# Alpha's products taken for two units at once, the first loads, scores and low halves in another order: a fused linear-attention and two-MoE kernel on one core

## The reference

```python
def _attn_ref(q, k, v, alpha):                 # (4, 8, 768, 48) each
    for t in range(S):
        state = alpha[:, :, t, :, None] * state + np.einsum('bhd,bhe->bhde', k[:, :, t], v[:, :, t])
        y[:, :, t] = np.einsum('bhd,bhde->bhe', q[:, :, t], state)

x = attn_out.transpose(0, 2, 1, 3).reshape(3072, 384)
h = x @ w_in1;  x = (h * (1.0 / (1.0 + np.exp(-1.702 * h)))) @ w_out1     # 384 -> 2048 -> 384
h = x @ w_in2;  x = (h - np.tanh(h)) @ w_out2
```

## Time and profile before

| what | value |
|---|---|
| median of 3 runs | 967.76 us (967.51 to 970.03) |
| profiled execution | 967.3 us, its span 965.5 us |
| PE busy | 943.8 us (98%) |
| DVE busy | 672.2 us (70%) |
| ACT, POOL busy | 376.4 us (39%), 285.4 us (30%) |
| granted TensorE clock | 1.00 in every stretch looked at |

### The profile page before, as it was taken

The page is one execution under the profiler, slowest core; times in us unless marked ns, Lnnn a source line. Parts: engine busy times, 40 slices in busy tenths (PEclk is TensorE's granted clock), DMA queues, the critical chain, the costliest instruction groups (busy, mean ns, idle before and its releaser), DMA issues.

```text
span 965.5 us, 23370 instructions
## 1 busy us (share of the span) xinstructions
PE 943.8 (98%) x9705; PEld 830.0 (86%) x9705; DVE 672.2 (70%) x1615; ACT 376.4 (39%) x730; POOL 285.4 (30%) x314
## 2 busy tenths in 40 slices
PE   5899999999999999999999999999999999999998
PEld 4789999999999988888888888888888888888886
DVE  7879997878888877776322544357677677776765
ACT  1352333332332332333234664244444444444442
POOL 2666665646556554444001642000000000000000
PEclk9999999999999999999999999999999999999999
DMA  7943232423323332321113322010020020100101
GB/s 156 256 89 91 49 86 51 114 49 85 80 61 83 90 69 47 104 47 25 19 58 123 98 82 90 1 37 30 1 66 2 1 66 1 40 27 1 34 1 33
DMA packets 136234, 58.94 MB, mean 61 GB/s; under 512 B 114368, under 2 KB 131520, under 8 KB 136128
## 3 DMA queue, kind: packets, MB, share of 16 engines
q1 hardware_dynamic: 133488, 55.39, 22.8%
q10 hardware_dynamic: 2640, 2.05, 0.7%
HBM read 43.26 MB, written 13.96 MB: 59 GB/s over the span
## 4 chain that ended last, share of the span: by engine, by line
PE 92%; DVE 3%; DMA 2%; SPq 1%; POOL 1%; issue 1%; ACT 0%; DVEq 0%; POOLq 0%; ACTq 0%
PE pX L840 39%; PE pZ L864 16%; PE pX L864 9%; PE pZ L908 6%; PE pZ L914 6%; PE pX L908 4%; PE pX L704 3%; PE pZ L799 2%; PE pZ L732 2%; PE pZ L690 1%; PE pZ L742 1%; DMA k<-k_t 1%; PE pX L835 1%; PE pX L718 1%; PE pZ L790 1%; DVE scores L1212 1%
## 5 line engine op out<-in xcount | busy, mean ns | idle before, releaser
L840 PE MATMUL pX<-x_hi,w_hi 128*128 128x512 f32 (+2 forms) x624 | 227.7, 365 | 0.7 <-ACT g L1050 0.7
L840 PE MATMUL pX<-x_lo,w_hi 128*128 128x512 f32 (+2 forms) x624 | 227.3, 364 | 0.0
L840 PE MATMUL pX<-x_hi,w_lo 128*128 128x512 f32 (+2 forms) x624 | 227.3, 364 | 0.0
L1228 DVE TENSOR_TENSOR g_lo<-g,g_hi 128x512 fp32r<-128x512 f32 (+2 forms) x208 | 129.3, 637 | 87.5 <-ACT g_hi L1059 87.3
L1059 ACT ACTIVATE g_hi<-g 128x512 fp32r<-128x512 f32 (+2 forms) x208 | 121.3, 583 | 89.5 <-DVE g L1308 85.9
L1050 ACT ACTIVATE g<-pX 128x512 f32<-128x512 f32 (+3 forms) x144 | 65.7, 456 | 206.4 <-PE pX L840 173.2
L1308 DVE TENSOR_TENSOR g<-pX,sg 128x512 f32<-128x512 f32 x96 | 66.3, 690 | 106.2 <-ACT sg L1052 106.2
L840 PEld LDWEIGHTS pX<-x_hi,w_hi 128*128 128x128 f32 x624 | 117.5, 188 | 18.0 <-ACT g L1050 1.1
L840 PEld LDWEIGHTS pX<-x_lo,w_hi 128*128 128x128 f32 x624 | 117.5, 188 | 16.9
L840 PEld LDWEIGHTS pX<-x_hi,w_lo 128*128 128x128 f32 x624 | 117.5, 188 | 16.8
L596 POOL TENSOR_TENSOR r<-r,alpha 112x128 f32<-112x128 f32 (+2 forms) x115 | 109.5, 968 | 18.5 <-DMA r<-q_t 14.9
(11 more groups left out here) (166 smaller groups left out, 1899.4 us busy)
## 6 DMA issues: line engine op xcount, KB each, us to landing
v<-v_l SPq DMA_DIRECT2D x96, 48.0 KB, 2.6
x_raw<-hidden SPq DMA_DIRECT2D x6, 768.0 KB, 5.7
attn_out<-y SPq DMA_DIRECT2D x92, 48.0 KB, 1.8
out_t<-o SPq DMA_DIRECT2D x10, 384.0 KB, 3.5
alpha<-a_t SPq DMA_DIRECT2D x24, 128.0 KB, 2.9
r<-q_t SPq DMA_DIRECT2D x24, 128.0 KB, 3.0
k<-k_t SPq DMA_DIRECT2D x24, 128.0 KB, 3.0
w_raw<-w_in SPq DMA_DIRECT2D x16, 192.0 KB, 2.4
```

The costliest lines, as they stand in the source:

```text
L840: last = nc.tensor.matmul(pH(N)[:, 0:w], win(wp, f, m), XS[T % 2][xp][:, m, 0:w], start=(n == 0), stop=(n == len(terms) - 1))
L1228: nc.vector.tensor_tensor(at(GLs, N), g_raw(N), at(GHs, N).bitcast(F32), ALU.subtract).then_inc(gl_done, 1)
```

## The change

It does the following.

- Alpha, SF1, T4, T16, F4, F16 and T64 hold two units side by side. `product_step` now does units 1 and 2, then 3 and 4, and so on in one pass (12 instructions of twice the size; unit 0 and, at the end, 23 alone), and `ahead` skips the alpha steps at every second odd item. Alpha's loads have a semaphore for each buffer and SP issues two units' alpha at once.
- In the opening, SP issues unit 1's alpha before the masks and unit 2's alpha before v of unit 0; ACT issues the g = 0 weights only after unit 1's q has landed; `first_inputs` is dealt out differently between SP and ACT, both starting with the first copy of y; ACT's `plain_queries(1)` comes after them. Unit 2's q and k go before both g = 1 weights; the g = 3 out weights go after unit 3's q and k. `first_unit` does alpha's first eight steps before any query. One warm-up product fewer.
- The up products 1 and 3 write bank O0 instead of H0, so a product need not wait for the gelu of the one before it, and the first `down` waits until four gelus are through (`g_done` 4) and the first states are copied.
- Visits stand at 0, 5, 9, 13, 17, 21, 25, 30, 33, 36, 40, 44, 47, 50, ... instead of 0, 4, 8, 12, 16, 20, 25, 30, 33, 36, 39, 42, 45, 49, 52, 55, 58, 61, ...; both lists go on with 64. Below N = 32 `plain_queries` comes after the visit's copies, not one N before.
- The low halves of w_out are one a period from N = 30 to 45. `x_low(2)` stands in the visit at N = 25, before its `ahead`.

```diff
 def batch_of(U):        return (U + 1) // 2
 def batch_end(U):       return min(2 * batch_of(U), UNITS - 1) + 1
...
-    starts = ([0, 4, 8, 12, 16, 20, 25, 30] + [33 + 3 * n for n in range(5)] + [49 + 3 * n for n in range(5)]
+    starts = ([0, 5, 9, 13, 17, 21, 25, 30, 33, 36, 40, 44, 47, 50, 53, 55, 58, 61]
...
 X_AT = {1: 13, 3: 12}
+XLOW_AT = {1: 9}
...
         def pH(N):
+            if N in (1, 3):
+                return O0
             return H0 if N < L1B * NF or N % 2 == 0 else H1
...
             def load_alpha(U):
-                if U:
-                    sp.wait_ge(t_step, (U - 1) * T_STEPS + T_AL)
-                    sp.wait_ge(q_step, (U - 1) * Q_STEPS + Q_AL)
+                if U > 1:
+                    sp.wait_ge(t_step, batch_of(U - 2) * T_STEPS + T_AL)
+                    sp.wait_ge(q_step, (U - 2) * Q_STEPS + Q_AL)
...
             load_k(sp, 0, 0)
+            load_alpha(1)
             sp.dma_start(MASK[:], masks).then_inc(mask_loaded, 16)
+            load_qk(1)
+            load_alpha(2)
             load_v(0)
-            load_alpha(1)
-            load_qk(1)
...
+                if U == 2:
+                    load_w(sp, 3, slice(1, 2))
                 if U == 1:
                     sp.wait_ge(y_copied, 1)
-                    first_inputs(sp, ((0, 0), (0, 1), (1, 0), (1, 1)))
+                    first_inputs(sp, ((0, 0), (1, 0)))
                 sp.wait_ge(y_copied, 2 * U)
                 if U == 1:
-                    first_inputs(sp, ((2, 0), (3, 0)))
+                    first_inputs(sp, ((2, 1), (3, 1)))
...
                 if U == 1:
-                    load_alpha(2)
-                    load_w(sp, 1, slice(1))
                     load_qk(2)
-                    load_w(sp, 1, slice(1, 2))
+                    load_w(sp, 1)
...
-                if U + 2 < UNITS:
-                    load_alpha(U + 2)
+                for W in (U + 2, U + 3):
+                    if U % 2 and W < UNITS:
+                        load_alpha(W)
                 if U == 1:
-                    load_w(sp, 3)
+                    load_w(sp, 3, slice(1))
...
                 if N < L1N:
-                    if N:
-                        pe.wait_ge(g_done, N)
+                    if N > 1:
+                        pe.wait_ge(g_done, N if N > 4 else N - 1)
...
                 if T < PLAIN:
-                    pe.wait_ge(g_done, N + 1)
+                    pe.wait_ge(g_done, max(4, N + 1))
...
+                if N == 0:
+                    pe.wait_ge(state_step, states_before(LEAD))
...
             plain_queries(0)
+            act.wait_ge(q_loaded[1], 32)
             load_w(act, 0)
-            plain_queries(1)
             copy_outputs(0)
+            act.wait_ge(y_copied, 1)
+            first_inputs(act, ((0, 1), (1, 1)))
             copy_outputs(1)
             act.wait_ge(y_copied, 2)
-            first_inputs(act, ((2, 1), (3, 1)))
+            first_inputs(act, ((2, 0), (3, 0)))
+            plain_queries(1)
...
-            queries_at = {VISIT_OF[j + 1] - 1: j // 2 + 1 for j in range(LEAD, ITEMS - 2, 2)}
+            queries_at = {VISIT_OF[j + 1] - (VISIT_OF[j + 1] >= L1P): j // 2 + 1 for j in range(LEAD, ITEMS - 2, 2)}
...
                 U = (j + 3) // 2 if j % 2 else j // 2 + 1
-                if U >= UNITS:
+                if U >= UNITS or j % 2 and U % 2 == 0:
                     return
...
             late = {NF + 1 + F: [(0, F)] for F in range(NF)}
-            for F in range(10):
-                late[NF + 6 + F].append((1, F))
-            late.update({2 * NF + 1: [(1, 10), (1, 11)], 2 * NF + 2: [(1, 12), (1, 13)], 2 * NF + 4: [(1, 14), (1, 15)]})
+            for F in range(NF):
+                late.setdefault(2 * NF - 2 + F, []).append((1, F))
...
                         states(j)
+                        if XLOW_AT.get(T) == f:
+                            x_low(T + 1)
                         ahead(j, 0)
```

More of the change, by code:

```diff
@@ L110, in made, with batch_of, batch_end @@
     return item_of(j)[3] < CHUNKS - 1
+def batch_of(U):
+    return (U + 1) // 2
+def batch_end(U):
+    return min(2 * batch_of(U), UNITS - 1) + 1
 def keys_before(j):
@@ L243, in build @@
         V = [sb(f"v_{u}", [P, 2, QP, D], where=att) for u in U2]
-        T64 = [sb(f"t64_{u}", [PX, SL], where=att) for u in U2]
+        T64 = sb("t64", [PX, 2 * SL], where=att)
         Y = [sb(f"y_{u}", [PX, 2, QP, C], where=att) for u in U2]
[L246 to L251, removed]
+        AL = sb("alpha", [PX, 2 * SL, C], where=att)
+        SF1 = sb("sf1", [PX, 2 * SL, C], where=att)
+        T4 = sb("t4", [PX, 2 * SL, 4, 4], where=att)
+        T16 = sb("t16", [PX, 2 * SL, 4], where=att)
+        F4 = sb("f4", [PX, 2 * SL, 8, 4], where=att)
+        F16 = sb("f16", [PX, 2 * SL, 8], where=att)
         S = sb("state", [PX, 2, SL, D], where=att)
@@ L376, in load_rows, with part_of, alpha_count @@
                 eng.dma_start(part, rows[at:at + (HS, D)[h]]).then_inc(done, 16)
+        def part_of(U):
+            n = (U + 1) % 2
+            return slice(n * SL, (n + 1) * SL)
+        def alpha_count(U):
+            return 32 * batch_of(U)
         def load_a(eng, U, half=None):
-            load_rows(eng, AL[:].rearrange("p (s t) -> p s t", s=SL), aT, U, al_loaded, half)
+            load_rows(eng, AL[:, part_of(U), :], aT, U, al_loaded[U % 2] if U else al0_loaded, half)
         def load_q(eng, U, half=None):
@@ L1049, in _ @@
                 if T < L1B:
-                    nc.scalar.activation(g_raw(N), H0[:, 0:width(T)], ACT.Gelu_apprx_sigmoid).then_inc(g_done, 1)
+                    nc.scalar.activation(g_raw(N), pH(N)[:, 0:width(T)], ACT.Gelu_apprx_sigmoid).then_inc(g_done, 1)
                 else:
@@ L1097, in product_step @@
             def product_step(U, s):
-                a, sf1 = ([t[:].rearrange("p (c s b) -> p c s b", s=4, b=16)[:, :, d, :] for d in range(4)]
-                          for t in (AL, SF1))
+                both = slice(part_of(U).start, part_of(batch_end(U) - 1).stop)
+                a, sf1 = ([t[:, both, d * 16:(d + 1) * 16] for d in range(4)] for t in (AL, SF1))
+                t4, f4 = T4[:, both, :, :], F4[:, both, :, :]
+                t16, f16 = T16[:, both, :], F16[:, both, :]
                 def after(steps):
-                    dve.wait_ge(t_step, U * T_STEPS + steps)
+                    dve.wait_ge(t_step, batch_of(U) * T_STEPS + steps)
                 def copy(out, src):
@@ L1110, in product_step @@
                 if s == 0:
-                    dve.wait_ge(al_loaded, (U + 1) * 32)
                     if U:
+                        for W in range(U, batch_end(U)):
+                            dve.wait_ge(al_loaded[W % 2], alpha_count(W))
                         dve.wait_ge(k4_ready, U)
+                    else:
+                        dve.wait_ge(al0_loaded, 32)
                     mul(sf1[1], a[2], a[3])
@@ L1186, in states @@
                         nc.vector.scalar_tensor_tensor(
-                            out=S[:, (ch + 1) % 2, s, :], in0=S[:, ch % 2, s, :], scalar=T64[U % 2][:, s:s + 1],
+                            out=S[:, (ch + 1) % 2, s, :], in0=S[:, ch % 2, s, :], scalar=T64[:, part_of(U).start + s:part_of(U).start + s + 1],
                             in1=pP[:, 2 * z + q, :], op0=ALU.mult, op1=ALU.add).then_inc(state_step, 1)
@@ L1315, in mul @@
                     nc.vector.tensor_tensor(out, in0, in1, ALU.mult).then_inc(q_step, 1)
-                for s in range(3):
+                for s in range(8):
                     product_step(0, s)
@@ L1327, in first_unit @@
                 dve.wait_ge(k_loaded[0], 32)
-                nc.vector.tensor_tensor(K4[0][:], K1[0][:], SF1[:], ALU.mult).then_inc(k4_ready, 1)
+                nc.vector.tensor_tensor(K4[0][:], K1[0][:], SF1[:, part_of(0), :].rearrange("p c t -> p (c t)"), ALU.mult).then_inc(k4_ready, 1)
                 dve.wait_ge(q_step, 4)
                 mul(r.qd4[:, :, 2:4, :], r.slot[:, :, 4:7:2, :], r.al[:, :, 0:1, :].to_broadcast([PX, SL, 2, SLOT]))
-                for s in range(4, 8):
-                    product_step(0, s)
                 key_step(0, 0)
@@ L1418, in _ @@
                     w_sums_low(k - 1)
-                if f == x_at(T) and PLAIN <= T + 1 < ALLB:
+                if f == x_at(T) and T not in XLOW_AT and PLAIN <= T + 1 < ALLB:
                     x_low(T + 1)
```

62 lines of the change are left out of this document (31 added, 31 removed).

## The result

The changed kernel takes **974.58 us** (median of 4 runs, 971.5 to 975.17) against 968.89 for the kernel before beside it (967.51 to 970.03): a ratio of 1.0057, with a 95% interval of 1.0041 to 1.0072. By that ratio it is 5.5 us slower, outside the predicted range. The profiled execution took 971.5 us, its span 969.7: 4.2 us more than the span before.

| piece | forecast | found |
|---|---|---|
| opening, up to the first product on x | +0.8 | +2.1 |
| first products | -3.0 | -1.4 |
| PE stands at 40 us | (none) | +3.2 |
| PE at the low clock behind it | (none) | +1.7 |
| stall at 55 us | -2.2 | -2.3 |

The account below looks back on a forecast made before the run. PE, busy 943.8 of 965.5 us, bounds the kernel, so only its idle time can go. 0.8 - 3.0 - 2.2 + 0.4 = -4.0 us gives 963.3 profiled, 963.7 us median; range 960.6 to 966.3.

Parts of the forecast that it names:

- That the first ninth decides, and the long middle stays: Whole program: PE's idle time that the change can touch lies before 107.4 us (16.5 us); the long middle has 1.2.
- The opening: Up to the first product on x: v lands near 16.5 us, behind weights and alpha 2; net 0.8 us later.
- my own list: Signs of being wrong: v after 18 us, PE wait over 1 us between 35 and 75, over 2 at N = 33.
- Rival 1: Opening: v lands in time, -0.7 us instead of +0.8, no wait at N = 33; 961.7 us in all; chance 0.22.
- The first products: First ups and scores of item 2: gelu waits go and scores start earlier, 3.0 us less.
- rival 4: First products: DVE was not the reason, gain 1.1 us instead of 3.0; 965.6 us; chance 0.22 together with rival 2.
- The stall at 55 us: PE's wait for ACT's copy of the keys goes, as the queries' copy comes after and keys come earlier: 2.2 us less.
- DVE at N = 25: N = 25 to 36: DVE idles before x_lo, PE waits about 1.2 us more at N = 33; net 0.4 us more.
- What stood at nothing: Parts counted as zero: fewer alpha passes, two units' alpha at once, masks and weights arriving before use, one warm-up fewer, later visits.
- Rival 2: A new wait at a later item, or v 2 us late, takes 2.2 us: 965.9; chance 0.22 together with rival 4.

Follow-up runs that it names:

- The three edits: Changed kernel with v of unit 0 ahead of alpha 2, group 2 weights behind alpha 3, low inputs of block 2 at slot 13: 962.48 us, again 963.24.

## Why the prediction was wrong

- **That the first ninth decides, and the long middle stays**: right. DVE's relief is worth nothing there (27 us less work, not the 17 I estimated).
- **The opening**, +0.8: the step that failed is "the 1.57 MB take 4.0 us: from about 10 to 14", and with it "v lands near 16.5". The weights' pieces moved from 10.6 to 16.7 us, with alpha 2 among them, and v landed at 18.5, which my own list said would make it wrong. What I had read in the earlier trace rows, that a queue issued later gets nothing for a while, did hold for v: its first piece moved 4.6 us behind its issue. (By the two lists of SP's DMAs v stands behind eight more, not ten; the sum doesn't use it.) The Trainium skill (DMA: Bandwidth & Descriptors, Queues, rings and completion order) has each engine take a packet in turn from the queues that have work. The traces don't show even turns: 457 packets of SP beside 621 of ACT from 12 to 15 us in one profile, 150 beside 726 in the other. What I drew from that rule, that v would be there in time, did not come about. Rival 1 (v in time) describes the kernel with v first: -1.2 us found, against its -0.7.
- **The first products**, -3.0: the visit after down 0 and up 5 came 10.05 us behind the first product (36.82 - 26.77); before, the same work was done after 34.80 + 1.34 - 24.70 = 11.44. That is 1.4. The step that failed is "six products take 4.0 and PE is there at 32.8". It left out four small waits: 0.36 and 0.22 us for ACT's copies of the keys, 0.52 for w_in of group 1, and 0.43 for instructions, 1.5 us in all. DVE started on the scores at 31.30 us, 0.4 behind the start of PE's last product for them, nearly as forecast, and PE did not wait for them. But 1.4 is nearer to rival 4's 1.1 than to my 3.0, and the run with the old visits shows that DVE's relief alone doesn't end the wait; so the number doesn't decide against rival 4. w_in was sent at 27.91 instead of 24.09: SP ended the first inputs 2.5 us later, and q and k of unit 2 stand ahead of it now in place of alpha 2.
- **The stall at 55 us**, -2.2: right, by the mechanism given, 2.3 us in the trace; alone, the line gave 1.7 us in the medians. The k that comes earlier may do the same (the run with the weights of groups 2 and 3 first), which isn't shown by itself.
- **DVE at N = 25**, +0.4: the mechanism was right (DVE idle 2.66 us ahead of x_lo, scores 15.8 us after the visit at N = 25 against 15.3 to 15.9 forecast), the size was 0.9 in the first profile, 28.4 - 27.5, and 2.6 in the second, 30.1 - 27.5, with the low clock, over my end of 2.5. DVE's scores are late twice in all in the earlier trace rows, not "twice more"; the 0.6 us near 107 are read rightly, and they went.
- **What stood at nothing**: PE's stop at 40 us and its low clock, 4.9 us together, are the step that turned the sign. "The masks and the weights g = 1 to 3 arrive before their use" looked only at what the program waits for, and nothing in the sum has a price for what these transfers hold up. My list had the sign for it, a wait of PE of over 1 us between 35 and 75 us; it was 3.0. PE's instructions use the same engines and have no line in the program. The Trainium skill (Runtime: NRT & Kernel Launch, Instruction fetch mechanics) says that an engine's sequencer fetches the next 16 KB while it works through the present ones, and that the cost is mostly hidden. The traces agree on the 16 KB, and for the kernel before on the rest; in the changed kernel the cost was 3.0 us and the low clock behind it. Rival 2 (a new wait takes the gain) was right in kind, but was priced at 2.2 us, the size of the gain that it was to cancel; nothing bounds a new wait by that.

Without the last point the profiled execution would have come to 971.5 - 4.9 = 966.6 us, 0.7 under the one before: no change that can be measured. With v in time as well (3.3 us, from the run with v first), it would have been at 963.3. That this is the forecast's own sum is chance: the forecast has v 1.1 us late in it, and its 3.0 us for the first products were 1.4.

## What to carry over

A change that moves bulk transfers earlier or later moves them against PE's instruction stream too: look at the instruction queues in the DMA view next to each burst, and at waits marked "issue". Here 0.11 MB of small rows moved beside 0.93 MB of large ones in 3 us, and v, issued behind the weights, mostly behind them; send what the first dependent step needs ahead of any wait in the same queue, not behind a prefetch. Price a new wait by what stands behind it, the clock included, not by the gain that it may cancel. And before a low clock is put down to a wait, look at a second profile of the same program.

## What the runs showed of the chip

- PE's instructions come in pieces of 16 KB over the DMA engines, one for about 250 matmuls and weight loads. Nearly all take 0.9 to 1.5 us; PE went on 1.3 to 1.6 us after the piece had landed, where it stood for one. With weights and alpha moving ahead of it (1.6 MB from 36 to 40.4 us), PE stood for 3.0 to 3.6 us in the four profiles with v late and the weights ahead of alpha 4. At which moment PE asks is not shown.
- PE's clock did not answer to the length of a wait alone. Around the wait for v it was at the lower level for nearly 7 us in two profiles (waits of 4.2 and 4.9 us) and stayed at 1.00 in three others (4.5, 4.7 and 4.9 us). Behind the stop at 40 us it fell in all four profiles with 3.0 to 3.6 us, and not behind 2.2. Behind the wait at N = 33 it fell in three of six, for 3 to 4 us, with waits of 1.6 to 2.0 us in all six; there it cost 1.4 to 1.5 us (10.0 to 10.1 us from N = 33 to 36 instead of 8.6). The three edits had 0.72 in one execution and 1.00 in another from 28 to 34 us. This is part of the scatter of several us between executions of one kernel.
